# Hash-bucket attention and a routed MLP on one core: one tile of the first batch's tokens is routed, gathered and put through its expert ahead of the others

## The chip, the core and the metric

The kernel runs on one core of a Trainium2 chip, in one launch. The metric is the device time of the launch in microseconds (us), lower is better. In the text PE is TensorE, DVE is VectorE, ACT is ScalarE, POOL is GpSimd, and SP is SyncE, which here only issues transfers.

## What is computed

Three parts follow each other. Their inputs and outputs are f32.

```python
# attention: B, H, S, D = 2, 8, 768, 64; a key counts only if its 6 sign bits equal the query's
mask   = q_bucket[:, :, :, None] == k_bucket[:, :, None, :]
scores = where(mask, q @ k.T / 8, -1e9)
x      = softmax(scores) @ v              # -> x: N = 1536 tokens, 512 wide

# experts: each token goes to the one of E = 8 experts with the largest logit
logits = x @ w_gate + modality_bias[modality_id]
e_idx  = argmax(logits, axis=1)
for e in range(E):                        # w1[e]: 512 x 1024, w2[e]: 1024 x 512
    mask = e_idx == e
    out[mask] = gate_w[mask, None] * (maximum(x[mask] @ w1[e], 0) @ w2[e])

# last MLP: 512 -> 2048 -> 512 with softplus
return softplus(x @ w_in) @ w_out
```

How many tokens an expert gets depends on the data; the kernel must be right for any split.

## The kernel before

**Attention.** A *step* handles 128 queries of one head against all 768 keys, a *body* is 12 steps (two heads), and there are 8 bodies: body 0 and body 7 are written out on every engine, those between run in hardware loops (DVE also writes out body 4). Step u of a body does on PE the scores of step u + 2 (`scores`, L1183), a third of the values of an earlier group (`values`, L1208), at u = 1, 4, 7, 10 a fold of the finished group into the bank `ps7` (`fold_out`, L1219), and six transposes of the probabilities (L1195). DVE does the row maximum of step u + 2 (L848 with the read of its accumulator), at the fold steps the three operations of `normalise` (L864, L866, L869), and two subtractions `pTl` (L855) on what ACT has just rounded (L596). ACT also does the exponentials (L587). The order of each engine's work is written out by hand in these functions; engines meet at semaphores. POOL splits the next head's q, k and v (`split_qk`, `split_v`), SP loads heads and moves rows of bits. `x_ready` counts normalised groups of three steps, of 32; 16 of them are the first batch. `X` holds for each token and head 64 values and 8 partial logits; SP stores it to `x_rows` in DRAM (`store_x`).

**Routing.** After the last fold DVE adds the last partial logits and finds each token's expert (`onehot`, L939 to L944). PE ranks the tokens within their experts with small bf16 products of triangular and all-ones matrices (L1264 to L1272); DVE and POOL turn the ranks into a place, a tile and a lane; PE makes the source row of each sorted place (`source`, L1282) and its gate factor (L1287). POOL gathers 12 tiles of 128 rows from `x_rows` in sorted order with indirect transfers (L523); ACT multiplies by the gate (`gated`, L668), PE transposes (`turn_x`, L1298), DVE copies to `xT` (L1012). A table of tiles and tokens per expert is read into registers (L268).

**Experts.** Tiles of 128 tokens run expert by expert; a tile belongs to one expert, so partly filled tiles occur. In the loop a tile is split into a rounded part and a rest, as are the weights, and each product is three fp32r products: `w1_products` (24 matmuls of 512 columns, L1323), `turn_h` (8 transposes), `turn_y` (4, of the tile before), `w2_products` (24 of 512 columns, L1343 to L1347). Weights lie in a ring of two slots (`RING`); SP loads the next expert's w1 when the first layer of the last tile before it is done (`hB_done`), w2 when its second layer is (`y_done`). The first tile of all takes its first layer in plain f32 (`first_products`, L1305: 32 matmuls of 128 columns), since its split weights are not there yet:

```python
turn_x(0); first_products()
for n in range(1, TPB + 1): turn_x(n)
w2_products(0, 0)
for n in range(TPB + 1, TILES): turn_x(n)
for e in range(E):
    with nc.tensor.Fori(0 if e else 1, n_e) as i:
        w1_products(e, g); turn_h(g, 0); turn_y(g - 1); turn_h(g, 1); w2_products(e, g)
```

The last MLP follows and isn't touched.

## Time and profile before

| | us |
|---|---|
| median of 3 runs | 764.47 (763.66 to 765.12) |
| the profiled execution's own time | 764.26 |
| its span | 762.5 |
| PE / DVE / ACT / POOL busy | 727.0 / 573.2 / 499.1 / 316.3 |

Attention takes the first 251 us of the span, routing and the start of the experts last to 291, the loop over the expert tiles to 490, and the last MLP takes the rest. Busy shares count matmuls whose ends are modelled, so PE's 95% says only that it is seldom without an instruction. In the rows below L12 is line 12 of the kernel before; `x4` counts instructions in a row that were merged, and the bracket at a row's end tells how long the engine had been idle and what released it.

### The profile page before, as it was taken

The numbers are of one execution on the slowest core, as the hardware profiler recorded it, in microseconds if no ns is written. First come the engines' busy times: TensorE is split into PE (matmuls) and PEld (weight loads), VectorE is DVE, ScalarE is ACT, GpSimd is POOL, SyncE is SP. The second block draws the span as 40 slices with busy tenths as digits, with TensorE's granted clock in tenths as the row PEclk, the third lists the DMA queues.
The fourth block names the chain that finished last, engine by engine and source line by source line (L and its number), as shares of the span: only waits on it lengthen the run. The fifth ranks groups of instructions, "written<-read, shape, count | busy, mean of one in ns | idle before, by whom it ended". The sixth has DMA issues, their size and how long they took to land. (4 is left out here: it accounts for less than half of the span.)

```text
span 762.5 us, 13117 instructions
## 1 busy us (share of the span) xinstructions
PE 727.0 (95%) x3974; PEld 619.8 (81%) x3974; DVE 573.2 (75%) x915; ACT 499.1 (65%) x914; POOL 316.3 (41%) x277
## 2 busy tenths in 40 slices
PE   5999999999999399999999999999999999999996
PEld 4899898998999287888888888878887888878884
DVE  6989999999998566427996254298787888887884
ACT  6878888788887355527985363375656665666662
POOL 7767577666742440000000000055554745457543
PEclk9999999999999689999999999999999999999999
DMA  3763111311101242306896001033322433324321
GB/s 132 276 198 123 41 46 38 129 56 48 36 5 69 72 141 110 111 0 240 327 361 230 0 0 28 3 97 94 110 83 97 152 103 90 104 89 149 99 70 69
DMA packets 38879, 80.52 MB, mean 106 GB/s; under 512 B 5536, under 2 KB 9792, under 8 KB 38848
## 3 DMA queue, kind: packets, MB, share of 16 engines
q1 hardware_dynamic: 36208, 72.82, 28.9%
q0 software_dynamic: 1920, 6.69, 2.7%
q10 hardware_dynamic: 720, 0.64, 0.2%
q8 instruction: 15, 0.25, 0.1%
q14 instruction: 16, 0.13, 0.1%
HBM read 72.33 MB, written 6.68 MB: 104 GB/s over the span
## 5 line engine op out<-in xcount | busy, mean ns | idle before, releaser
L529 POOL TENSOR_TENSOR hres<-hexp,hres 128x512 f32<-128x512 f32 x46 | 59.7, 1297 | 320.1 <-DVE hres L1081 320.0
L596 ACT ACTIVATE pTh<-psA 128x384 fp32r<-128x384 f32 x192 | 83.9, 491 | 41.4 <-PE psA L1195 40.9
L855 DVE TENSOR_TENSOR pTl<-psA,pTh 128x384 fp32r<-128x384 f32 x192 | 97.9, 551 | 11.0 <-ACT pTh L596 9.7
L1183 PE MATMUL psA<-K,Q 128*128 128x384 f32 x384 | 93.2, 366 | 3.2 <-ACT K L633 1.6
L848 DVE TENSOR_SCALAR_CACHE_REDUCE psA<-psA 128x768 f32<-128x768 f32 x96 | 91.8, 957 | 3.4 <-PE psA L1183 3.4
L587 ACT ACTIVATE probs<-psA,negmax 128x768 f32<-128x768 f32 x96 | 87.4, 910 | 2.9 <-DVE psA L848 2.5
L1019 DVE SCALAR_TENSOR_TENSOR hTl<-psA,hTh 128x512 fp32r<-128x512 f32 x34 | 22.8, 689 | 87.5 <-ACT hTh L687 87.5
L1035 DVE TENSOR_TENSOR wil<-rawi,wih 128x512 fp32r<-128x512 f32 x48 | 79.1, 1650 | 6.5 <-ACT wih L707 6.5
L1195 PE MATMUL psA<-ident,probs 128*128 128x128 f32 x576 | 82.6, 279 | 1.1 <-DVE pTl L855 0.5
L765 ACT ACTIVATE habs<-psA 128x512 f32<-128x512 f32 x48 | 28.7, 597 | 77.8 <-PE psA L1396 77.8
L1195 PEld LDWEIGHTS psA<-ident,probs 128*128 128x128 f32 x576 | 65.0, 144 | 14.5 <-issue 5.9
L532 POOL TENSOR_TENSOR hsum<-hsum,hres 128x512 f32<-128x512 f32 x46 | 69.6, 1513 | 8.2 <-POOL hres L529 8.2
L1410 PE MATMUL psA<-woh,sh 128*128 128x512 f32 x184 | 72.2, 392 | 0.9 <-DVE sl L1098 0.7
L1412 PE MATMUL psA<-woh,sl 128*128 128x512 f32 x184 | 71.7, 390 | 0.0
L1411 PE MATMUL psA<-wol,sh 128*128 128x512 f32 x184 | 71.7, 389 | 0.0
L1183 PEld LDWEIGHTS psA<-K,Q 128*128 128x128 f32 x384 | 64.3, 195 | 6.2 <-issue 5.3
L1208 PE MATMUL ps<-pTh,vhl 128*128 128x384 f32 x186 | 62.7, 337 | 0.0
L1208 PE MATMUL ps<-pTl,vhl 128*128 128x384 f32 x186 | 62.6, 336 | 0.0
L1343 PE MATMUL ps<-w2h,hTh 128*128 128x512 f32 x136 | 54.9, 404 | 0.0
L1098 DVE TENSOR_TENSOR sl<-hsum,sh 128x512 fp32r<-128x512 f32 x47 | 53.6, 1141 | 0.9 <-ACT sh L779 0.9
L1344 PE MATMUL ps<-w2l,hTh 128*128 128x512 f32 x136 | 53.2, 391 | 0.0
L1396 PE MATMUL psA<-x2h,wih 128*128 128x512 f32 x192 | 51.7, 391 | 0.7 <-DVE hsum L1089 0.6
(185 smaller groups left out, 1653.5 us busy)
## 6 DMA issues: line engine op xcount, KB each, us to landing
w2s<-in_moe_w SPq DMA_DIRECT2D x8, 2048.0 KB, 9.3
w1s<-in_moe_w SPq DMA_DIRECT2D x8, 2048.0 KB, 9.4
rawi<-in_moe_w_in SPq DMA_DIRECT2D x48, 256.0 KB, 2.7
rawo<-in_moe_w_out SPq DMA_DIRECT2D x48, 256.0 KB, 2.8
raw<-in_qk SPq DMA_DIRECT2D x16, 384.0 KB, 3.1
vs<-in_v SPq DMA_DIRECT2D x16, 192.0 KB, 2.4
x_rows<-X SPq DMA_DIRECT2D x1, 1728.0 KB, 6.0
x_rows<-X SPq DMA_DIRECT2D x1, 1512.0 KB, 5.5
```

The source lines that it names most:

```text
L532: pool.tensor_tensor(hsum[u][:, :], hsum[u][:, :], hres[u][:, :], ALU.add).then_inc(s_done, 1)
L587: nc.scalar.activation(probs[u % 2][:, :].rearrange("p (a n) -> p a n", a=2), psA[u % 2][:, :, 0:HALF], ACT.Exp, bias=negmax[:, u % 4:u % ...
L596: nc.scalar.activation(pTh[u // TPGR % 2][:, g * TPH:(g + 1) * TPH, u % TPGR * P:(u % TPGR + 1) * P], psA[2][:, g, 0:HALF].rearrange("p (t ...
L848: V.tensor_scalar(psA[u % 2][:, :, 0:HALF], psA[u % 2][:, :, 0:HALF], PENALTY, PENALTY, ALU.min, ALU.min, accum_out=negmax[:, u % 4:u % 4 ...
L855: V.tensor_tensor(pTl[u // TPGR % 2][:, g * TPH:(g + 1) * TPH, cols], psA[2][:, g, 0:HALF].rearrange("p (t n) -> p t n", t=TPH), pTh[u // ...
L1035: V.tensor_tensor(wil[u][:, :, :], rawi[u][:, :, :], wih[u][:, :, :].bitcast(F32), ALU.subtract).then_inc(wi_split, 1)
L1183: last = T.matmul(psA[u % 2][:, h, 0:HALF], qs[par][:, cols], ks[par][:, h * HALF:(h + 1) * HALF], start=start, stop=not start)
L1195: last = T.transpose(psA[2][:, g, t * P:(t + 1) * P], probs[u % 2][:, kt * P:(kt + 1) * P], ident[:, :])
L1208: last = T.matmul(last_ps if type(G) is int and G == PAIRS - 1 else ps6[:, 0:COLS], vhl[gm // 2 % 2][:, kt, :], p[gm % 2][:, kt, :], start ...
L1410: T.matmul(acc[t], sh[u][:, cols], woh[u][:, :], start=first, stop=False)
L1411: T.matmul(acc[t], sh[u][:, cols], wol[u][:, :], start=False, stop=False)
L1412: last = T.matmul(acc[t], sl[u][:, cols], woh[u][:, :], start=False, stop=final)
```

## The change

In body 6 (`choose`) DVE finds the experts of the first batch's 768 tokens, counts them with one matmul of PE and takes the expert with most of them, `favourite`, and its number of tokens, at most 128. In body 7 (`collect`) it ranks the favourite's tokens with two matmuls, picks the first 128, and PE makes their source rows with 12 more. POOL gathers them (`xin0`), after it has summed the first batch's logits between bodies 4 and 5. SP loads the favourite's weights into slot 1 of the ring, which held expert 1's before; expert 1's weights are now loaded after this tile's products. The tile (tile 0) goes through both layers in plain f32: its first layer in three pieces between the routing's small products, its second between the transposes of the other tiles. The 128 tokens leave the regular sort; the favourite has 128 fewer. The first regular tile (tile 1) is now the one with a plain f32 first layer. Body 6 is written out on PE and DVE.

```diff
 # PE, attention
+                    if type(j) is int and j == BODIES - 2 and u == 6:
+                        pe.wait_ge(counts0_ready, 1)
+                        pe.wait_ge(x_ready, j * 4)
+                        T.matmul(ps7[:, 0:E], ones_b[:, :], sums16[:, 0, :], start=True, stop=True).then_inc(counts0_done, 1)
+                    if last and u == 3:
+                        pe.wait_ge(member_ready, 1)
...
+                    if last and u == 8:
...
                     if u % TPGR == 1 and not (first and u < 7):
+                        if type(j) is int and j == BODIES - 2 and u == 7:
+                            pe.wait_ge(counts0_read, 1)
+                        if last and u == 4:
+                            pe.wait_ge(rank0_read, 1)
+                        if last and u == 10:
+                            pe.wait_ge(source0_ready, 1)
```

```diff
 # DVE, attention: between row_max and low_pT of a step
+                    if type(j) is int and j == BODIES - 2:
+                        choose(u)
+                    if last:
+                        collect(u)
...
+                    elif u == 4:
+                        dve.wait_ge(rank0_done, 1)
+                        V.tensor_copy(rank0[:, :], ps7[:, 0:TPB]).then_inc(rank0_read, 1)
+                        dve.wait_ge(rank0_read, 1)
+                        alone(V.scalar_tensor_tensor(taken0[:, :], rank0[:, :], float(P), member[:, :], ALU.is_lt, ALU.mult))
...
+                    elif u == 6:
+                        V.scalar_tensor_tensor(pick0[:, :, :], iota_p[:, :].unsqueeze(1).broadcast_to([P, TPB, P]), 1.0,
+                                               over(key0[:, :], P), ALU.add, ALU.is_equal).then_inc(pick0_ready, 1)
...
+                    elif u == 11:
+                        dve.wait_ge(gathered_first, 16)
+                        alone(V.tensor_reduce(logit0[:, :], xin0[:, :, D:XROW].rearrange("p h e -> p e h"), AX.X, ALU.add))
```

```diff
 # SP
-                if i < 2 + 2 * RING:
-                    (load_w2, load_w1)[i % 2](i // 2 - 1)
+                if i < 4:
+                    (load_w2, load_w1)[i % 2](0)
...
+            sp.wait_ge(table0_ready, 1)
...
+            sp.dma_start(w1s[1][:, :, :], w1[bass.ds(at, 1)].rearrange("o (c p) f -> p (o c) f", p=P)).then_inc(w1_in[1], 16)
+            sp.dma_start(w2s[1][:, :, :], w2[bass.ds(at, 1)].rearrange("o (c p) f -> p (o c) f", p=P)).then_inc(w2_in[1], 16)
...
-            for e in range(RING, E):
...
+            for e in range(1, E):
...
                 sp.wait_ge(hB_done, before_e)
                 load_w1(e)
```

```diff
 # PE, start of the experts
+            pe.wait_ge(xT0_ready, 1)
+            pe.wait_ge(w1_in[1], 16)
+            first_layer(range(0, 2), w1s[1], xT0)
             pe.wait_ge(onehot_ready, 1)
...
             T.matmul(total_ps[:, 0:E], ones_b[:, :], sums16[:, 0, :], start=True, stop=True).then_inc(totals_done, 1)
+            first_layer(range(2, 6), w1s[1], xT0)
...
             last.then_inc(source_done, 1)
+            first_layer(range(6, FC), w1s[1], xT0)
...
-            turn_x(0)
-            pe.wait_ge(w1_in[0], 16)
-            pe.wait_ge(xT_ready, 1)
-            first_products()
...
-            for n in range(1, TPB + 1):
+            pe.wait_ge(w2_in[1], 16)
+            for n in range(5):
+                second_layer((n,))
                 turn_x(n)
-            w2_products(0, 0)
-            for n in range(TPB + 1, TILES):
-                turn_x(n)
+            second_layer(range(5, FC))
+            pe.wait_ge(w1_in[0], 16)
+            pe.wait_ge(xTf_ready, 1)
+            for f in range(FC):
+                first_layer((f,), w1s[0], xTf)
+                if f + 5 < TILES:
+                    turn_x(f + 5)
+            turn_y(0)
+            w2_products(0, 1)
```

`first_layer` does for each f four f32 matmuls of 128 columns, `second_layer` one f32 matmul of 512 columns. The order of the instructions shows it at two places.

PE, from the last fold to the first gathered tile, before (L1219 is the fold, L1264 to L1272 the ranks and counts, L1282 the source rows, L1287 the gates, L268 the table, L1298 `turn_x`, L1305 the first layer):

```order
L1219 MATMUL ps<-foldg,oT_102 128x72 x3
L1264 MATMUL psA<-onehot,before_b 128x96
...
L1272 MATMUL psA<-sums,ones_b 128x8
L1282 MATMUL psA<-carry,pick 128x12 x24
L1287 MATMUL psA<-gates,pick 128x36 x12
L268 TENSOR_LOAD table x2
L1298 MATMUL psA<-ident,xs_117 128x128 x4
L1305 MATMUL psA<-xT,w1s_49 128x128 x32
L1298 MATMUL psA<-ident,xs_118 128x128 x4
```

The same place now:

```order
L1464 MATMUL psA<-ident,xs_121 128x128 x4
L1397 MATMUL ps<-foldg,oT_102 128x72 x3
L1472 MATMUL psA<-xT_122,w1s_50 128x128 x8
L1490 MATMUL psA<-onehot,before_b 128x96
...
L1498 MATMUL psA<-sums,ones_b 128x8
L1472 MATMUL psA<-xT_122,w1s_50 128x128 x16
L1509 MATMUL psA<-carry,pick 128x12 x24
L1472 MATMUL psA<-xT_122,w1s_50 128x128 x8
L1515 MATMUL psA<-gates,pick 128x36 x12
L298 TENSOR_LOAD table x2
L1482 MATMUL ps<-w2s_54,hT_123 128x512
L1526 MATMUL psA<-ident,xs_117 128x128 x4
```

The 32 matmuls of tile 0's first layer (`xT_122` is `xT0`, `w1s_50` the ring's slot 1) stand around the ranks and the source rows, ahead of all gathered tiles; behind the table now comes tile 0's second layer (L1482), one matmul between each two transposed tiles.

DVE, steps 3 and 4 of body 7, now (L933, L949 to L954 and L940 are the former L848, L864 to L869 and L855):

```order
L933 TENSOR_SCALAR psA,negmax<-psA 128x2x384
L940 TENSOR_TENSOR pTl_82<-psA,pTh_94 128x3x128 x2
L933 TENSOR_SCALAR psA,negmax<-psA 128x2x384
L1044 COPY rank<-ps 128x6
L1046 SCALAR_TENSOR_TENSOR taken<-rank,member 128x6
L949 TENSOR_SCALAR den<-sums 128x3
L951 RECIPROCAL inv<-den 128x3
L954 TENSOR_TENSOR X<-ps,inv 128x3x72
L940 TENSOR_TENSOR pTl_82<-psA,pTh_94 128x3x128 x2
```

L1044 and L1046 are new; they stand behind the row maximum, and PE's fold of the same step waits for L1044 to have read `ps7`.

## Rows read from the trace of the kernel before

**Rows 1.** Stretches: length, busy us per engine, clock, DMA share, GB/s
```profile
195.00:222.00 27.00, 26.94 (x191) 24.39 (x191) 25.36 (x57) 22.42 (x51) 17.21 (x15) 1.00 0.05 13
222.00:249.00 27.00, 26.14 (x184) 25.08 (x183) 23.30 (x59) 19.87 (x46) 6.17 (x16) 1.00 0.16 59
```

**Rows 2.** Timeline of DVE, bodies 6 and 7: start us, us, instruction
```profile
208.63 0.55 DVE L864 TENSOR_SCALAR den<-sums 128x3 f32<-128x3 f32 x1
...
221.56 1.02 DVE L855 TENSOR_TENSOR pTl<-psA,pTh 128x384 fp32r<-128x384 f32 x2 [0.20 <-ACT pTh L596]
...
223.37 0.17 DVE L864 TENSOR_SCALAR den<-sums 128x3 f32<-128x3 f32 x1
```

**Rows 3.** DVE's groups by shape, 249 to 264: busy us, mean ns
```profile
L963 DVE TENSOR_TENSOR pick<-iota_p,lane_f 128x640 bf16<-128x640 f32 x2 | 1.8, 937 | 0.0
...
L939 DVE TENSOR_TENSOR lg<-lg,X 128x48 f32<-128x48 f32 x1 | 0.2, 209 | 0.1
...
L959 DVE SCALAR_TENSOR_TENSOR lane_f<-tile_f,place_f 128x12 f32<-128x12 f32 x1 | 0.2, 174 | 0.0
```

**Rows 4.** Timeline, step 4 of body 7: row maximum and fold
```profile
229.08 0.96 DVE L848 TENSOR_SCALAR_CACHE_REDUCE psA<-psA 128x768 f32<-128x768 f32 x1
229.10 0.78 PE L1219 MATMUL ps<-foldg,oT 128*128 128x72 f32 x6
```

**Rows 5.** Timeline: end of POOL split, PE near it, logit sums
```profile
160.77 1.85 POOL L452 TENSOR_TENSOR K<-raw,K 64x768 fp32r<-64x768 f32 x1 [0.34 <-POOL K L449]
...
169.77 0.51 PE L1183 MATMUL psA<-K,Q 128*128 128x384 f32 x2
...
243.99 3.08 POOL L507 TENSOR_TENSOR lg<-lg,X 128x96 f32<-128x96 f32 x7
```

**Rows 6.** Timeline from the ranks to the first tile's first layer
```profile
253.59 0.22 PE L1264 MATMUL psA<-onehot,before_b 128*128 128x96 bf16 x1 [2.30 <-DVE onehot L944]
...
258.21 0.81 PE L1282 MATMUL psA<-carry,pick 128*128 128x12 bf16 x22 [3.69 <-POOL carry L516]
...
262.67 0.54 PE L1287 MATMUL psA<-gates,pick 128*128 128x36 bf16 x12 [3.06 <-DVE gates L986]
...
264.65 0.72 ACT L668 ACTIVATE xs<-xin,gate_at 128x512 f32<-128x512 f32 x1 [8.77 <-DMA xin<-x_rows,source]
...
267.42 9.75 PE L1305 MATMUL psA<-xT,w1s 128*128 128x128 f32 x64 [0.88 <-DVE xT L1012]
```

**Rows 7.** Stretches, columns as in rows 1
```profile
269.00:271.00 2.00, 2.00 (x12) 2.00 (x11) 2.00 (x2) 2.00 (x2) 1.70 (x2) 0.50 0.85 240
...
273.00:275.00 2.00, 2.00 (x21) 2.00 (x20) 1.09 (x2) 0.60 (x1) 1.69 (x2) 1.00 0.34 106
```

**Rows 8.** Timeline: the last 20 records of L1305
```profile
274.77 2.40 PE L1305 MATMUL psA<-xT,w1s 128*128 128x128 f32 x20
```

**Rows 9.** PE reads the table: ns min/median/max, first and last start
```profile
L268 PEldq TENSOR_LOAD <-table x2: 345/431/517, 262.7 to 263.3; - x2
```

**Rows 10.** First product of the regular tiles, as rows 9
```profile
L1323 PE MATMUL psA<-w1h,xth x128: 387/389/476, 291.4 to 481.1; 128*128 128x512 f32 x128
```

**Rows 11.** Timeline of PE, regular tiles: turns, second layer, starts of two tiles
```profile
296.98 0.60 PE L1332 MATMUL psA<-ident,hrow 128*128 128x128 f32 x4
297.42 0.60 PE L1355 MATMUL ps<-ident,yrow 128*128 128x128 f32 x4
...
298.32 0.50 PE L1343 MATMUL ps<-w2h,hTh 128*128 128x512 f32 x1
...
303.89 1.07 PE L1323 MATMUL psA<-w1h,xth 128*128 128x512 f32 x4
...
316.26 1.07 PE L1323 MATMUL psA<-w1h,xth 128*128 128x512 f32 x4
```

**Rows 12.** Timeline of POOL: issue of the last of 12 gathers
```profile
277.03 0.95 POOL L523 DMA_INDIRECT xin<-x_rows,source  x1 [0.30 <-issue]
```

**Rows 13.** Stretches while one w1 loads, columns as in rows 1
```profile
301.00:303.00 2.00, 2.00 (x11) 1.65 (x10) 1.08 (x2) 2.00 (x2) 0.00 (x0) 1.00 1.00 410
```

More of the change, by code:

```diff
@@ L140, in build @@
         xs = [work(f"xs{i}", [P, DM], 99328 + 2048 * i) for i in range(2)]
+        pick0 = work("pick0", [P, TPB, P], 101376, BF16)
+        xin0 = work("xin0", [P, H, XROW], 99072)
+        xs0 = work("xs0", [P, DM], 101376)
+        xT0 = work("xT0", [P, DC, P], 103424)
+        hT0 = work("hT0", [P, FC, P], 105472)
+        xTf = work("xTf", [P, DC, P], 133120)
         w2h = work("w2h", [P, FC, DM], 0, F32R)
@@ L171, in build @@
         lower = sb("lower", [P, TILES, E])
-        at8 = sb("at8", [P, TILES, E])
+        at9 = sb("at9", [P, TILES, E + 1])
+        tok = sb("tok", [P, TPB, 2], BF16)
+        later = sb("later", [P, TPB, TPB])
+        member = sb("member", [P, TPB], BF16)
+        ahead_of = sb("ahead_of", [P, TPB], BF16)
+        rank0 = sb("rank0", [P, TPB])
+        taken0 = sb("taken0", [P, TPB])
+        key0 = sb("key0", [P, TPB])
+        chosen = sb("chosen", [P, E])
+        most = sb("most", [P, 1])
+        code0 = sb("code0", [P, 1])
+        table0 = sb("table0", [P, 2], I32)
+        source0 = sb("source0", [P, 1], I32)
+        logit0 = sb("logit0", [P, E])
+        neg0 = sb("neg0", [P, 1])
+        sum0 = sb("sum0", [P, 1])
+        gate0 = sb("gate0", [P, 1])
         highest = sb("highest", [P, TILES])
@@ L720, in _, with take_h0 @@
             nc.scalar.activation(tmp8[:, :, :], tmp8[:, :, :], ACT.Exp).then_inc(gexp_done, 1)
-            act.wait_ge(source_ready, 2)
-            for n in range(2):
-                gated(n)
+            def take_h0(half, done):
+                act.wait_ge(done, 1)
+                nc.scalar.activation(hT0[:, half * FC // 2:(half + 1) * FC // 2, :],
+                                     psA[1][:, half, :].rearrange("p (c n) -> p c n", c=FC // 2), ACT.Relu).then_inc(hT0_ready, 1)
+            take_h0(0, hA_done)
+            w1_high(0, 0)
+            take_h0(1, hB_done)
             act.wait_ge(table_ready, 1)
@@ L1251, in _ @@
             body(0, first=True)
-            with nc.tensor.Fori(1, BODIES - 1) as j:
+            with nc.tensor.Fori(1, BODIES - 2) as j:
                 body(j)
+            body(BODIES - 2)
             body(BODIES - 1, last=True)
@@ L1299, in turn_x @@
                 last.then_inc(xT_done, 1)
[L1301 to L1310 removed]
             def w1_products(e, g):
[L1314 removed]
+                pe.wait_ge(xl_ready, g - 1)
                 for half, done in ((0, hA_done), (1, hB_done)):
```

306 lines of the change are left out of this document (222 added, 84 removed).

## The prediction, written before the change was timed

> **What bounds the kernel now.** I read three things in this order. First the busy time by stretch in attention: DVE is busy 25.4 of 27 us in body 6 and 23.3 of 27 at the end [rows 1], more than ACT or POOL; PE's figure is no measure, since its ends are modelled. Then DVE's timeline, to see whether the rest is slack: in a step without a fold DVE does the row maximum, waits 0.20 us for ACT's `pTh` [rows 2] and goes on; steps with a fold or with bits show no such wait. So in attention nearly each us that DVE gets is a us on the path, less a gap of 0.2 in about half the steps. Third the timeline behind attention: PE does its ranks at 253.6, waits 3.7 us for `carry`, 3.1 for `gates`, and starts the first tile's first layer at 267.4 only [rows 6]. Its granted clock is at 0.50 (the 1.2 GHz level) when that layer starts and back at 1.00 from 273 us [rows 7]. The regular tiles start at 291.4 [rows 10], one each 12.37 us (303.89 to 316.26) [rows 11], with no stall seen in PE's rows.
>
> **1. One tile less in the loop: -12.4.** L1323 has 128 matmuls of `xth`, 8 in a tile, so 16 tiles are in the loop behind the one that is peeled [rows 10]. Now tile 0 and tile 1 stand ahead of it. The count of tiles stays at 17 if the favourite has 128 tokens in the first batch: taking a full tile from an expert takes one off its tiles. Counting the reference's choices on its own inputs, experts have 177, 484, 91, 35, 81, 7, 386 and 275 tokens, that is 2, 4, 1, 1, 1, 1, 4 and 3 tiles; expert 1 has 247 in the first batch, so it is the favourite, 128 are taken and 356 (3 tiles) stay. The loop then has 15: 12.37 us less.
>
> **2. Attention: +6.8.** DVE gets 16 operations in body 6 and 14 in body 7. Prices by size, from DVE's groups [rows 3]: 0.17 for one of a few elements, 0.21 for 48, and the `pick0` of 768 columns 1.07 (0.94 for 640, scaled with a fixed share of 0.27). Body 6: six of about 0.21, one count of 0.25 and nine small, 3.0 us. Body 7: 3.5 us, of which `pick0` is 1.07. Sum 6.5.
> - Off, what falls into the 0.2 us gaps: steps 0, 5, 6, 8 and 11 of body 6 and two of body 7, and both operations of step 11, where DVE no longer has a row maximum: -1.6.
> - On, the port: L864, which is small, takes 0.55 where POOL works and 0.17 where it doesn't [rows 2]. Four such (`tensor_scalar` and a cast between SBUF tiles) stand in steps 7, 9 and 10 of body 6, with POOL at work near all three: +1.0 (0 to 1.5).
> - On, a new wait in step 4 of body 7: the fold of that step went out at 229.10, just as the row maximum began at 229.08 (0.96 long) [rows 4]; now it needs `rank0_read`, behind that maximum and the copy: about 230.25. PE's transposes, ACT's rounding and DVE's `pTl` of the step are queued behind it. Of these 1.15 us the 0.3 of DVE's two operations are counted above: +0.85.
> The sum is 6.75. Bounds: 3.7 if all of DVE's idle time in the two bodies took operations in, 9.5 if none did and the waits between dependent operations came on top.
>
> PE's own additions (1, 2 and 12 matmuls of at most 8 columns) are hidden by its wait for `pTl`: the 24 like them at L1282 took about 1 us [rows 6], so 12 take 0.5 in step 8, where DVE has 0.38 to do at once. The gather of `xin0`: `source0` is ready in step 8 near 239.7, and after the routing it took 4.9 us from the end of L1282 (258.21, its last two included about 259.7) to ACT's start at 264.65 [rows 6]; that makes 244.6, DVE asks for it at 244.9. Hidden, 0.3 us ahead; if it is late, its lateness goes 1:1 onto the last step. The gate, `xs0` and its transposes fall in ACT's and PE's waits for the last values: 0.
>
> POOL's new place for bias and sums holds up the split for head 11 by some 5.4 us: seven sums of 96 columns took 3.08 [rows 5], those of 48 are put at 2.5, bias and constants at 2.9. It ended at 162.6 and would end at 168.0; PE's scores near it stand at 169.77 [rows 5]. Hidden, by 1.5 us at most. SP now waits for `table0` in front of nothing but the favourite's loads and the last stores: 0. Both loads, asked for near 219, are there by 235: 2 MB at 410 GB/s [rows 13] are 5 us.
>
> **3. From the gates to the loop: +1.8.** The first layer of tile 0 goes into PE's waits: 8 matmuls from 251.3 to 253.2 (ranks at 253.6), 16 to 258.2 (source rows at 258.2), 8 to 261.5 (gates at 262.7). A plain f32 matmul of 128 columns is two records of 0.117 (2.40 us for 20, less the last one's tail) [rows 8], 0.235. So 0 for it, if the clock stays at 1.00; the same work at 0.50 is a rival below. From the gates on PE has: the table, read at 262.7 and 263.3, 0.5 at most each, and a third read [rows 9], ready at 264.3; 8 f32 matmuls of 512 columns, 0.90 each (between 2 x 0.43 by columns and 4 x 0.235): 7.2; 12 turns of 0.44 (296.98 to 297.42) [rows 11]: 5.3; tile 1's first layer, 32 x 0.235: 7.5; `turn_y` 0.44; its second layer, 5.45 (298.32 to 303.89 less a start of 0.1) [rows 11]. Together 290.2, and 0.5 for the first gathered rows, which come at the pace of POOL's issue: 290.7. Before it was 291.4, so -0.7.
>
> Transfers come on top. Expert 1's w1 no longer lies in the ring; SP asks for it as soon as tile 0's first layer is done, near 262, in the midst of the 12 gathers. Before, the gathers alone took 0.85 of the DMA engines at 240 GB/s [rows 7], and one w1 alone takes all of them at 410 GB/s [rows 13]. If both share evenly, a gather takes 2.0 us in place of 1.25 until w1 is in at 275: `turn_x(4)` then waits till 273.6, not 271.1, and w2, asked for when tile 0's second layer is done, slows the last ones, which have 3 us in hand. I take +2.5, between 0 (gathers lose nothing) and 10 (weights go first).
>
> The Trainium skill (DMA: Bandwidth & Descriptors, "Issuing engines are not separate DMA queues") says that transfers from all engines run on the same 16 DMA engines and interleave. No stretch before has a gather beside a weight load, so no row shows how they share; by the rule the sum is the one below, without it 2.5 less.
>
> Sum: 764.26 - 12.4 + 6.8 + 1.8 = 760.5, against the profiled execution; the median of the runs lies 0.2 above it: **760.7**.
>
> **Rivals.**
> - *The cover is better* (the gaps take DVE's operations in, or the gathers lose nothing). Either alone gives -3 or -2.5, both 764.3 - 12.4 + 3.7 - 0.7 = 754.9; I price it 757. For it: POOL's last gather goes out at 277.0 [rows 12], 4 us before PE needs it now. Against: rows 2 show no gap in half the steps.
> - *Weights go first; slower.* The 2 MB of w1 pass ahead of gathers 1 to 5, 5.0 us at 410 GB/s [rows 13], and w2 ahead of the last ones, 5.0 less what is in hand: some 9.5 in place of 2.5, so 767.5. It decides from a third term of +7.2 on. For it: a load keeps the engines full with what is queued at once, while POOL feeds gathers one by one. Against: before, the gathers finished a while after their issue without trouble.
> - *The clock stays down.* At 0.50 the 16 matmuls behind the counts take 7.5, not 3.8, and hold up the source rows by 3.7, and the last 8 the gates by 0.8: 765.0, no change to be measured. For it: before, PE's clock fell in that very stretch [rows 6, 7]. Against: it fell while PE had hardly anything to do, and now it is to be busy.
>   The Trainium skill (TensorE: Matmul & The Clock Gate, Part 1) says "the default state is throttled, and activity releases the throttle", which speaks against this rival; the return to 1.00 in rows 7 agrees, the outcome here is shown by no run yet.
> - *No tile is saved* (the count above is wrong): 764.5 + 6.8 + 1.8 = 773.1, with a chance of 0.04.
>
> **How the numbers follow.** What a measurement of this kernel can tell from no change is 0.2%, 1.5 us. Chances: the forecast 0.50 (758 to 763.5 by its own bounds, a sixth of it above 762.9 and so "same"), better cover 0.20, weights first 0.16, clock 0.10, no tile 0.04. Faster 0.42 + 0.20 = 0.62; same 0.08 + 0.10 = 0.18; slower 0.16 + 0.04 = 0.20. The range 756.5 to 767 leaves out the low end of the second case, half of the third and all of the last.
>
> **What would show it.** Term 1: 120 records of `xth` in `w1_products` in place of 128, still 12.4 us apart. Term 2: the last fold's normalise ends 6.8 us later than at 251.8; steps without new work keep their length; the fold of step 4 in body 7 starts behind the copy from `ps7`. Term 3: the gates' matmuls at the same distance from the last fold, clock 1.00 throughout; the distance from the gates to the loop 30.5 us in place of 28.7, with waits of PE or ACT for `xin` in it. If the distance is under 29, transfers cost nothing; above 35, the weights go first. The prediction is wrong as a whole if attention grows by under 3 or over 10 us, or if POOL's split of head 11 is what the scores wait for.

## The result: 756.5 us, and the profile after

| | before | after |
|---|---|---|
| median (runs) | 764.16 us (4) | 756.48 us (4; 754.92 to 756.95) |
| ratio to before | | 0.9894, 95% interval 0.9876 to 0.9912 |
| profiled execution, its span | 764.26, 762.5 us | 756.76, 755.0 us |
| last normalise of attention starts | 251.39 | 253.10: **+1.7** |
| from there to the products for the gates | 11.28 | 11.11: -0.2 |
| from those to the first regular tile | 28.74 | 32.19: **+3.45** |
| first to last product of the regular tiles | 189.7 | 177.3: **-12.4** |
| behind it | 281.4 | 281.3: -0.1 |

The last five rows add up to the 7.5 us between the spans. 760.7 was forecast, and the range began at 756.5: the change saved 4.2 us more than forecast, and the median lies 0.02 us outside the range. Five more runs of the changed kernel (e15, below) had a median of 754.36, all nine together 755.4, so it is outside by more than that. In e15's profile attention grew by 1.0 us and the stretch from the gates to the first regular tile by 2.0: the rows of this table are of single executions.

What answers to [rows 10], the first product of the regular tiles (columns as there):

```profile
L1540 PE MATMUL psA<-w1h,xth x120: 389/389/389, 296.4 to 473.7; 128*128 128x512 f32 x120
```

120 records in place of 128: one tile less, and term 1 of the prediction stands to a tenth of a us.

PE behind attention and one row of ACT, to be read against [rows 6] (start us, us, engine, line, ...):

```profile
252.83 2.00 PE L1472 MATMUL psA<-xT,w1s 128*128 128x128 f32 x16
254.99 0.22 PE L1490 MATMUL psA<-onehot,before_b 128*128 128x96 bf16 x1 [0.16 <-DVE onehot L1122]
...
255.80 3.82 PE L1472 MATMUL psA<-xT,w1s 128*128 128x128 f32 x32
259.63 0.81 PE L1509 MATMUL psA<-carry,pick 128*128 128x12 bf16 x22
...
264.21 0.47 PE L1515 MATMUL psA<-gates,pick 128*128 128x36 bf16 x12 [1.30 <-DVE gates L1164]
265.83 1.10 PE L1482 MATMUL ps<-w2s,hT 128*128 128x512 f32 x2 [1.15 <-issue]
...
271.01 0.72 ACT L738 ACTIVATE xs<-xin,gate_at 128x512 f32<-128x512 f32 x1 [4.27 <-DMA xin<-x_rows,source]
271.78 1.11 PE L1526 MATMUL psA<-ident,xs 128*128 128x128 f32 x4 [3.48 <-ACT xs L738]
```

The waits of 3.69 and 3.06 us of [rows 6] are filled by the early tile's first layer. But a new wait stands behind the gates: PE's transposes of the second gathered tile begin after 3.48 us of idling, because ACT waits 4.27 us for that tile's rows. The stretches around it (columns as in [rows 1]):

```profile
269.00:271.00 2.00, 0.00 (x0) 0.00 (x0) 1.22 (x2) 0.00 (x0) 1.70 (x2) 1.00 1.02 411
271.00:273.00 2.00, 1.22 (x5) 1.22 (x6) 0.07 (x1) 1.16 (x2) 1.39 (x3) 0.64 1.04 404
273.00:275.00 2.00, 2.00 (x5) 0.86 (x5) 1.75 (x2) 1.53 (x3) 1.69 (x2) 0.51 1.04 394
275.00:277.00 2.00, 2.00 (x11) 1.22 (x10) 1.69 (x2) 1.05 (x2) 1.52 (x2) 1.00 0.96 302
```

The DMA engines are full until 275 (share 1.02 to 1.04, some 400 GB/s), and PE's granted clock, which had stayed at 1.00 through the routing, falls to 0.51 (the 1.2 GHz level) behind PE's idle stretch. What PE does from 271.78 to 275.11 (four transposes, two matmuls, four transposes) took 1.79 us in e1, at 1.00, and takes 3.33 here.

Attention grew by 1.7 us only. DVE in body 6, where 16 operations came in, and POOL's operation beside it:

```profile
207.09 2.12 POOL L465 TENSOR_SCALAR qs<-raw 64x768 f32<-64x768 f32 x1
208.61 0.63 DVE L1015 TENSOR_SCALAR chosen<-totals,most 128x8 f32<-128x8 f32 x1
208.74 0.51 DVE L949 TENSOR_SCALAR den<-sums 128x3 f32<-128x3 f32 x1
...
213.88 0.16 DVE L1019 TENSOR_REDUCE code<-chosen 128x1 f32<-128x8 f32 x1
213.96 0.14 DVE L1020 TENSOR_SCALAR most<-most 128x1 f32<-128x1 f32 x1
214.02 1.01 DVE L940 TENSOR_TENSOR pTl<-psA,pTh 128x384 fp32r<-128x384 f32 x2
```

Two things are to be seen. The three operations that don't wait for each other start 0.06 to 0.08 us apart, though the two small ones last 0.14 and 0.16. And the long one (0.63) ends at 209.24 with POOL's, which ran from 207.09 to 209.21; the existing `den` behind it, which had waited 0.55 in [rows 2], ends at the same time. The wait was met once, not twice.

Body 7, with PE's fold of step 4:

```profile
230.07 0.16 DVE L1044 COPY rank<-ps 128x6 f32<-128x6 f32 x1
...
230.29 0.89 PE L1397 MATMUL ps<-foldg,oT 128*128 128x72 f32 x6 [0.94 <-DVE rank L1044]
...
231.29 0.38 DVE L954 TENSOR_TENSOR X<-ps,inv 128x216 f32<-128x216 f32 x1 [0.56 <-PE ps L1397]
232.07 1.02 DVE L940 TENSOR_TENSOR pTl<-psA,pTh 128x384 fp32r<-128x384 f32 x2 [0.40 <-ACT pTh L659]
...
235.95 0.95 DVE L1051 SCALAR_TENSOR_TENSOR pick<-iota_p,key 128x768 bf16<-128x768 f32 x1
```

The fold of step 4 waits 0.94 us for the copy of the ranks, as forecast, and the selection matrix `pick0` takes 0.95.

### The profile page after: what moved, and what is told of

The parts are those of the page before. It is cut to its first block and busy times, and to the rows that moved or that the text cites. A ratio compares the mean times of both kernels' runs of the same rounds, so it can differ in the third digit from the quotient of the medians.

```text
span 755.0 us, 13130 instructions
## 1 busy us (share of the span) xinstructions
PE 726.8 (96%) x4017; PEld 618.0 (82%) x4017; DVE 573.3 (76%) x944; ACT 500.1 (66%) x916; POOL 318.3 (42%) x288
## 5 line engine op out<-in xcount | busy, mean ns | idle before, releaser
L659 ACT ACTIVATE pTh<-psA 128x384 fp32r<-128x384 f32 x192 | 83.9, 491 | 42.9 <-PE psA L1373 42.3
L940 DVE TENSOR_TENSOR pTl<-psA,pTh 128x384 fp32r<-128x384 f32 x192 | 97.8, 551 | 10.7 <-ACT pTh L659 9.6
L933 DVE TENSOR_SCALAR_CACHE_REDUCE psA<-psA 128x768 f32<-128x768 f32 x96 | 91.8, 956 | 2.6 <-PE psA L1361 2.5
L1560 PE MATMUL ps<-w2h,hTh 128*128 128x512 f32 x128 | 51.7, 404 | 0.0
L1617 PE MATMUL psA<-x2l,wih 128*128 128x512 f32 x192 | 51.4, 389 | 0.0
```

The lines of the kernel that those rows point to most:

```text
L659: nc.scalar.activation(pTh[u // TPGR % 2][:, g * TPH:(g + 1) * TPH, u % TPGR * P:(u % TPGR + 1) * P], psA[2][:, g, 0:HALF].rearrange("p (t ...
L933: V.tensor_scalar(psA[u % 2][:, :, 0:HALF], psA[u % 2][:, :, 0:HALF], PENALTY, PENALTY, ALU.min, ALU.min, accum_out=negmax[:, u % 4:u % 4 ...
L940: V.tensor_tensor(pTl[u // TPGR % 2][:, g * TPH:(g + 1) * TPH, cols], psA[2][:, g, 0:HALF].rearrange("p (t n) -> p t n", t=TPH), pTh[u // ...
L1617: last = T.matmul(hps[u], w[u][:, d, :], x[:, d, g * GTOK:(g + 1) * GTOK], start=first, stop=(w is wil and d == DC - 1))
```

## The experiments

Since single spans scatter by 1 us and more, each run is read in two ways: the median and its ratio to the kernel before on the same chip, and distances inside the profiled execution, which repeat to 0.07 us where nothing was touched (body 6 of the changed kernel: 29.34 to 29.41 in the nine runs that leave it and the bodies ahead of it alone). *Body 6* is the distance from its first row maximum to that of body 7; *body 7* from there to the last normalise of attention (the row maximum stands two steps ahead of its own step, in all kernels); *gates to loop* as in the table above.

| kernel | median us | ratio to before, interval | body 6 | body 7 | gates to loop |
|---|---|---|---|---|---|
| before | 764.16 | | 29.62 | 31.05 | 28.74 |
| changed | 756.48 | 0.9894 (0.9876 to 0.9912) | 29.39 | 32.69 | 32.19 |
| e15: changed, again | 754.36 | 0.9880 (0.9864 to 0.9896) | 29.37 | 32.70 | 30.76 |
| e1: load behind the gathers | 752.16 | 0.9853 (0.9836 to 0.9870) | 29.36 | 32.69 | 27.64 |
| e2: ranks in step 3 | 754.74 | 0.9878 (0.9864 to 0.9893) | 29.37 | 31.96 | 32.13 |
| e3: before, body 6 written out | 762.70 | 0.9985 (0.9976 to 0.9993) | 29.27 | 31.04 | 28.50 |
| e4: 16 products more | 762.24 | 0.9978 (0.9966 to 0.9991) | 36.33 | 34.85 | 31.04 |
| e5: 16 maxima more | 759.35 | 0.9938 (0.9924 to 0.9951) | 31.64 | 33.71 | 32.31 |
| e6: DVE's bodies written out | 756.26 | 0.9886 (0.9870 to 0.9901) | 29.47 | 32.68 | 33.38 |
| e7: `pick0` on POOL | 754.72 | 0.9880 (0.9865 to 0.9895) | 29.34 | 32.67 | 30.79 |
| e8: e1, first layer behind the gates | 759.20 | 0.9930 (0.9917 to 0.9944) | 29.36 | 32.71 | 35.46 |
| e9: e1 + e2 | 751.30 | 0.9830 (0.9817 to 0.9844) | 29.35 | 32.02 | 27.66 |
| e10: e9 + bodies written out | 751.10 | 0.9829 (0.9816 to 0.9842) | 29.43 | 31.98 | 27.65 |
| e11: e9 + `pick0` on POOL | 752.44 | 0.9843 (0.9829 to 0.9856) | 29.36 | 32.25 | 27.64 |
| e12: all four | 750.93 | 0.9826 (0.9812 to 0.9839) | 29.46 | 32.10 | 28.54 |
| e13: e9, only the copy in step 3 | 751.95 | 0.9836 (0.9823 to 0.9849) | 29.41 | 31.48 | 29.19 |
| e14: e13 + bodies written out | 750.35 | 0.9817 (0.9804 to 0.9829) | 29.44 | 31.49 | 28.57 |
| e16: before, bodies written out | 762.75 | 0.9976 (0.9966 to 0.9986) | 29.28 | 31.07 | 28.52 |

### e1: does the load of expert 1's w1 hold up the gathers?

```diff
                 sp.wait_ge(hB_done, before_e)
+                if e == 1:
+                    sp.wait_ge(gathered[TILES - 1], 16)
                 load_w1(e)
```

> The changed kernel, but SP asks for expert 1's w1 only when the last of the 12 gathers has landed. Theory (the loads share the DMA engines with the gathers, and this is what the second gathered tile waits for): in the changed kernel ACT waits 4.27 us for xin at 271.0, PE 3.48 us behind it, and PE's clock falls to 0.51 to 0.64 for 2 to 3 us behind that wait. All this goes: gates to loop 28 to 28.5 us in place of 32.2, so 3.5 to 4.5 us faster than the changed kernel, near 752.4. Rival (the gathers land late by themselves, since rows are scattered or POOL issues them slowly): gates to loop stays within 0.5 us of 32.2 and the time is the same. Second rival (the load is only moved, to where its wait is met again, at expert 1's first tile): gathers early, but a wait of ACT for w1 in the loop, no gain.

27.64 us from gates to loop, and 4.3 us off the median against the first four runs of the changed kernel (2.2 against e15's, where the intervals of the ratios still touch; the 3.1 to 4.5 us between the profiles carry the reading). The stretch in e1 (columns as in [rows 1]), and PE there:

```profile
269.00:271.00 2.00, 2.00 (x8) 0.77 (x6) 2.00 (x4) 1.07 (x2) 1.70 (x2) 1.00 0.80 221
271.00:273.00 2.00, 1.76 (x9) 0.95 (x9) 2.00 (x3) 1.71 (x3) 1.54 (x2) 1.00 0.70 212
```
```profile
272.77 0.63 PE L1528 MATMUL psA<-ident,xs 128*128 128x128 f32 x4 [0.24 <-DVE xT L1192]
```

The wait of 3.48 is gone, the clock stays at 1.00, and the loads, now asked for at 281.7 and 282.1, are there long before expert 1 begins (ACT splits its w1 at 300.4 with no wait). The theory holds, both rivals fall. Of the 4.5 us between the two profiles, 3.5 are the wait and 1.5 the slower clock behind it, less the shorter waits that e1 has. How the two shared the DMA engines shows in the queues of the changed kernel (q1 is SP's load, q0 POOL's gathers: packets, MB, share), first from 265 to 267 us, then from 269 to 271; the last row is e1's from 265 to 267, without the load:

```profile
q1 hardware_dynamic: 175, 0.72, 87.8%
q0 software_dynamic: 34, 0.08, 11.2%
```
```profile
q1 hardware_dynamic: 104, 0.43, 52.5%
q0 software_dynamic: 106, 0.40, 49.8%
```
```profile
q0 software_dynamic: 113, 0.38, 71.2%
```

For the first 4 us the load took seven parts in eight (from 267 to 269 it was 171 packets against 29), then half. The gathers had more to move: POOL had begun to send off three by 265, as in e1, where 113 packets of theirs passed in the same 2 us. The Trainium skill (DMA: Bandwidth & Descriptors, "Queues, rings and completion order") says that a DMA engine takes turns between the queues it has work for, a packet at a time. The second stretch agrees with that, 104 packets against 106; the first doesn't, 175 against 34.

### e2, e9 and e13: the new wait in step 4

```diff
-                    elif u == 4:
+                    elif u == 3:
                         dve.wait_ge(rank0_done, 1)
                         V.tensor_copy(rank0[:, :], ps7[:, 0:TPB]).then_inc(rank0_read, 1)
```

The comparison `taken0` behind the copy moves with it. In e13, which has e1's edit too, it goes back to step 4 and only the copy stays.

> The changed kernel, but DVE reads the ranks from PSUM in step 3 of body 7, not in step 4. Theory (the fold of step 4 waits for that read, and all queued behind it on PE): the fold starts near 229.2 in place of 230.29, the last normalise of attention ends 0.8 to 1.2 us earlier, the time is 0.8 to 1.2 us below the changed kernel. Rival (the step waits for ACT or the row maximum anyway, and the late fold is caught up): less than 0.3 us. Second rival (the read in step 3 waits for PE's rank product, which ends near 227.25, and delays that step): slower by 0.1 to 0.5.

> The changed kernel with both edits at once: expert 1's w1 asked for behind the gathers (e1), and the ranks read in step 3 (e2). Alone they gave 4.3 us and 1.7 us of medians against the changed kernel, of the latter 0.75 us inside body 7. Theory (two separate stretches, nothing shared): 0.6 to 1.5 us faster than e1, so 750.7 to 751.5. Rival (the gates come earlier but the gathers don't, and PE waits for them): the same as e1, 752.2.

> e9, but only the copy of the ranks out of PSUM stands in step 3; the comparison of 6 columns behind it goes back to step 4. In e2, e9 and e10 that comparison took 1.00 to 1.02 us in step 3, since it began within 0.01 us of POOL's split of V (227.98 and 227.97 in e9) and ended with it. Theory (that wait is what it costs): the comparison takes 0.16 to 0.2 us, attention ends 0.6 to 0.9 us earlier than in e9, near 750.6. Rival (step 3 has slack, or ACT's pTh ends last there): within 0.2 us of e9, 751.3.

From row maximum to row maximum, steps 3 and 4 of body 7 took 2.11 and 2.63 us before, 2.18 and 3.81 in the changed kernel, 2.94 and 2.50 in e2, 2.14 and 2.66 in e13. So the late fold had cost 1.18 us. e2 took it away and paid 0.76 of it again, for an operation on 6 columns: body 7 is 0.73 us shorter, just under the 0.8 to 1.2 of its theory, and its median, 754.74, lies between the two of the changed kernel, so as a time it shows nothing. e9 is 0.9 us below e1, as its theory has it, with runs that overlap. Here is the comparison in e9, with POOL's operation:

```profile
227.97 1.01 POOL L510 TENSOR_TENSOR vhl<-vs,vhl 128x384 fp32r<-128x384 f32 x1 [0.18 <-POOL vhl L508]
```
```profile
227.78 0.16 DVE L1046 COPY rank<-ps 128x6 f32<-128x6 f32 x1
227.98 1.02 DVE L1048 SCALAR_TENSOR_TENSOR taken<-rank,member 128x6 f32<-128x6 f32 x1
228.93 1.01 DVE L942 TENSOR_TENSOR pTl<-psA,pTh 128x384 fp32r<-128x384 f32 x2
```

The comparison began 0.01 us behind POOL's split of V and ended with it. In e13 the comparison takes 0.16:

```profile
229.46 0.16 DVE L1049 SCALAR_TENSOR_TENSOR taken<-rank,member 128x6 f32<-128x6 f32 x1
229.54 0.16 DVE L951 TENSOR_SCALAR den<-sums 128x3 f32<-128x3 f32 x1
```

Body 7 is 0.54 us shorter than in e9, near the forecast of 0.6 to 0.9. The median isn't: 751.95 against 751.30. e13's profile lost 1.5 us from gates to loop, 1.14 of it in one wait of PE for a gathered tile. The local theory holds; as a time, e13 is no gain over e9.

### e3 and e16: what does a loop cost DVE?

```diff
-            with nc.vector.Fori(BODIES // 2 + 1, BODIES - 1) as j:
+            with nc.vector.Fori(BODIES // 2 + 1, BODIES - 2) as j:
                 body(j, 1)
+            body(BODIES - 2, 1)
             body(BODIES - 1, 1, last=True)
```

> The kernel before, but DVE's body 6 is written out behind the loop, as the changed kernel has it, with no new operation in it. Theory (in a loop the column of X that a fold's normalise writes comes from a register, and DVE starts that instruction 0.14 to 0.28 us later behind the reciprocal than with a constant: 0.34 to 0.46 us from start to start in body 6 of before, 0.21 in the changed kernel; four folds): 0.7 to 1.1 us faster than before, so that 16 small operations of body 6 in the changed kernel cost about 0.7 us and not 0. Rival (the gap behind the reciprocal is slack, since ACT's pTh comes no sooner): within 0.2 us of before, and then the 16 operations are free.

> The kernel before with all of DVE's bodies 1 to 6 written out, and nothing else. Theory (a register in the address of a fold's normalise delays it by 0.14 to 0.28 us, four times in a body; body 6 alone gave 1.46 us of medians, 0.5 of it in its own profile): 2 to 4 us faster than before, 760.5 to 762.5. Rival (body 6 alone has all of the gain, the rest is hidden behind ACT and PE): 762.5 to 763.

A fold's last operations in body 6, before (first fence) and in e3:

```profile
201.83 0.18 DVE L866 RECIPROCAL inv<-den 128x3 f32<-128x3 f32 x1
202.17 0.38 DVE L869 TENSOR_TENSOR X<-ps,inv 128x216 f32 x1 [0.16 <-DVE inv L866]
```
```profile
201.43 0.17 DVE L866 RECIPROCAL inv<-den 128x3 f32<-128x3 f32 x1
201.64 0.38 DVE L869 TENSOR_TENSOR X<-ps,inv 128x216 f32<-128x216 f32 x1
```

In the loop, with a register in the address, 0.34 us pass from start to start here and 0.34 to 0.46 in the four folds of the body; written out, with a constant, 0.21. (The edit takes the whole loop away; that it is the address isn't shown apart.) Body 6 becomes 0.35 us shorter, less than the 0.8 of the four gaps together, so part of them had been slack. The median is 1.46 us lower (the ratio 0.15%), more than the profile shows inside the body, and the rest of it isn't explained here. With all bodies written out (e16) the median is no lower than with one, 762.75, where 2 to 4 us had been forecast; the ratios, 0.9976 against 0.9985, leave room for some 0.7 us. What this says of the changed kernel: its body 6 is written out too, and 29.39 against e3's 29.27 is the net price of its 16 operations: **0.13 us** (0.06 to 0.14 over the runs that repeat either body).

The rows of the two traces show where the rest went. Six of the 16 stand in fold steps, ahead of a `den` that waits for POOL anyway: from the end of the row maximum to the end of `den` the four folds take 2.6 us in e3 and 2.8 in the changed kernel. The other ten filled most of DVE's waits for ACT's `pTh`: 1.19 us in e3's body 6, 0.14 in the changed kernel's.

### e4 and e5: 16 operations more

Behind each operation of `choose` one more, on constants, into a tile that nobody reads; e4 a product, e5 a maximum. The edit of e5:

```diff
+                for n in range({6: 2, 9: 2, 10: 3}.get(u, 1)):
+                    alone(V.tensor_reduce(spare[n][:, :], first_tile(by_tile(iota_e[:, :])), AX.X, ALU.max))
```

> The changed kernel with 16 more small DVE operations in body 6: behind each that chooses the expert one product of 48 columns on constants, into a tile that nobody reads (the kernel's outputs don't change). Theory (a small operation that doesn't wait for the one ahead starts 0.06 to 0.12 us behind it, and the wait for the port that POOL shares is met once in a step whatever the number): +1.0 to +1.9 us. Rival as in the prediction (0.21 us each, and more where POOL works): +3.4 us or more. Second rival (the steps have slack): under 0.4 us.

> The changed kernel with 16 more small DVE operations in body 6 at the same places as in e4_double_small, but maxima of 48 into 6 columns in place of products (into tiles that nobody reads, the outputs don't change). In e4 DVE's products that began while POOL ran an operation ended with it, up to 1.81 us later. Theory (what an added operation costs is 0.1 us from start to start, less the slack of its step; the 5.8 us of e4 were waits for the end of POOL's running operation, which a maximum over columns doesn't make): +0.2 to +1.5 us against the changed kernel, and none of the added maxima longer than 0.25 us. Rival (any operation shifts the steps against POOL's and the existing ones then wait): +3 us or more, with the waits in the operations that were there. Second rival (fixed price of 0.2 us each): +3.2 us with no long operation.

e4's body 6 grew by 6.9 us, twice the 3.4 at which its dearest case began, body 7 by 2.2, and the median by 5.8 to 7.9. The longest wait in it, POOL and DVE:

```profile
202.31 1.82 POOL L492 TENSOR_TENSOR Q<-qs,Q 64x768 fp32r<-64x768 f32 x1 [0.18 <-POOL Q L489]
```
```profile
202.38 1.81 DVE L1005 TENSOR_TENSOR onehot<-first,red 128x48 bf16<-128x48 f32 x1
```

The operation that waited longest was none of the added ones, but an operation of the change, moved to where POOL had just begun (added products waited too, one for 0.88 us at 199.78). In e5 no added maximum waited: alone they take 0.19 to 0.25 us. Through step 9, with 12 of them, e5's row maxima fell back by 0.33 us against the changed kernel, 0.03 each. Then this:

```profile
216.08 1.82 POOL L492 TENSOR_TENSOR Q<-qs,Q 64x768 fp32r<-64x768 f32 x1 [0.18 <-POOL Q L489]
```
```profile
216.24 1.68 DVE L950 TENSOR_SCALAR den<-sums 128x3 f32<-128x3 f32 x1
```

In the changed kernel `den` of that step began 0.17 us ahead of the same operation of POOL and took 0.15; here it begins 0.16 behind it. Step 10 grew by 1.6 us with it, and the five behind it by 1.4 more, in part waits of DVE for ACT (0.68 in the first of body 7); the median is 2.9 to 5.0 us up. So my theory for e5 (that kinds of operation which don't wait would settle it) falls, and its rival holds: it matters where the existing ones end up. The Trainium skill (SBUF — State Buffer, "SBUF: two separate sides") has the rule: DVE and GpSimd share a pair of ports that is an exclusive lock. A GpSimd operation takes it, and so does a DVE operation in a two-port mode or with two inputs in SBUF; the one that starts first has it for its whole instruction, and the other is blocked. Each pair of rows here agrees, with ends within 0.1 us of each other (204.13 and 204.19; 217.90 and 217.92; 228.98 and 229.00).

### e6, e10, e12, e14: DVE's bodies 1 to 5 written out

```diff
-            with nc.vector.Fori(1, BODIES // 2) as j:
-                body(j, 0)
-            body(BODIES // 2, 1)
-            with nc.vector.Fori(BODIES // 2 + 1, BODIES - 2) as j:
-                body(j, 1)
+            for j in range(1, BODIES - 2):
+                body(j, 1 if j >= BODIES // 2 else 0)
```

> The changed kernel with DVE's bodies 1 to 5 written out too, so that DVE has no loop in attention and no register in an address or a wait there. Writing out body 6 alone made the kernel before 1.46 us faster (0.35 of it seen inside that body). Theory (each body in a loop costs 0.35 to 1.1 us more): -1.8 to -5 us against the changed kernel, that is 751.5 to 754.7. Rival (what e3 gained was a shift in the start of attention that differs from build to build): within 1 us of the changed kernel. Second rival (the longer program is fetched more often and DVE waits for code): slower.

> e9 with DVE's bodies 1 to 5 written out as well. In e6 attention ended 1.5 us earlier than in the changed kernel, and the distance from the gates to the loop was 33.4 us in place of 32.2, so that nothing was left of it; there the gathers shared the DMA engines with the load. Theory (the loss was the load's; without it attention's gain stays): 0.5 to 1.5 us faster than e9. Rival (what attention gained was its early start, which differs from execution to execution by 0.5 to 0.9 us, and writing out bodies 1 to 5 gains nothing): within 0.4 us of e9.

> e11 with DVE's bodies 1 to 5 written out as well: all four edits. Theory (they add): 0.5 to 1.5 us faster than e11, near 749.5. Rival: as for e10, within 0.4 us of e11.

> e13 with DVE's bodies 1 to 5 written out. Theory (the two add, and bodies 1 to 5 give what the profiles of e6, e10 and e12 showed, 1.4 us): 1.0 to 1.6 us faster than e13, near 749.3. Rival (medians of e6 and e10 stood only 0.2 below their counterparts): within 0.4 us of e13.

Against their counterparts the medians moved by -0.2 (e6, first runs) or +1.9 (e6, e15's), -0.2 (e10), -1.5 (e12) and -1.6 us (e14); in the profiles body 6 began 0.8 to 1.6 us earlier in all four. Two things are mixed in that. From the first row maximum of body 1 to that of body 6 it is 147.0 to 147.4 us in all kernels with loops and 146.3 to 146.5 in the five without (e16 too): 0.7 to 1.0 us are the loops'. Where body 1 begins scatters from 42.9 to 44.0 whatever the kernel, and the rest is that. In the medians the gain shows in e12 and e14 and not in e6 and e10, so as a time it is likely but not certain. Behind the gates PE's clock fell to 0.50 in e12 (265 to 267) and e14 (264 to 266), with no load beside the gathers: e12's stretch to the loop is 0.9 us longer than e11's, e14's is 0.6 shorter than e13's, which had waited for a gathered tile. e14 has the lowest median of the study; its interval overlaps those of e9, e10 and e12.

### e7 and e11: the selection matrix on POOL

```diff
 # POOL
+            pool.wait_ge(key0_ready, 1)
+            for t in range(TPB):
+                pool.tensor_scalar(pick0[:, t, :], iota_p[:, :], 1.0, key0[:, t:t + 1],
+                                   ALU.add, ALU.is_equal).then_inc(pick0_ready, 1)
...
 # DVE, step 6
-                        V.scalar_tensor_tensor(pick0[:, :, :], iota_p[:, :].unsqueeze(1).broadcast_to([P, TPB, P]), 1.0,
-                                               over(key0[:, :], P), ALU.add, ALU.is_equal).then_inc(pick0_ready, 1)
```

> The changed kernel, but the selection matrix of the early tile is built by POOL in 6 pieces of 128 columns, not by DVE in one operation of 0.95 us in step 6 of body 7. Theory (POOL is idle there and DVE is on the path): step 6 shrinks by 0.65 us, the last normalise of attention ends 0.5 to 0.7 us earlier. Rival (POOL's pieces of about 0.6 us each, 3.6 in all, come too late for PE's product in step 8, and PE waits, or DVE's small operations wait for them): 0 to 2 us slower.

> e9 with the selection matrix built by POOL in 6 pieces, as in e7, but from ranks that are there a step earlier. In e7 step 6 became 0.65 us shorter, and steps 8 and 9 longer by 0.5, since POOL's pieces took 4.24 us and PE's product of step 8 came late. Theory (a step more of room hides POOL's pieces): 0.4 to 0.9 us faster than e9. Rival (DVE's small operations of the fold in step 4 or 7 then meet POOL at work and wait for its piece, 0.7 us at a time): within 0.3 us of e9, or slower.

In e7 step 6 went from 2.75 to 2.11 us, and steps 7 and 8 from 2.51 and 2.00 to 2.63 and 2.40: body 7 is unchanged (32.67). e7's rows say why:

```profile
233.56 4.24 POOL L564 TENSOR_SCALAR pick<-iota_p,key 128x128 bf16<-128x128 f32 x6 [5.09 <-DVE key L1052]
239.28 0.45 PE L1426 MATMUL ps<-tok,pick 128*128 128x1 bf16 x12
240.16 0.88 ACT L663 ACTIVATE pTh<-psA 128x384 fp32r<-128x384 f32 x2 [0.65 <-PE psA L1375]
240.68 1.02 DVE L944 TENSOR_TENSOR pTl<-psA,pTh 128x384 fp32r<-128x384 f32 x2 [0.32 <-ACT pTh L663]
```

POOL's pieces end at 237.80, 1.5 us before PE's 12 products of step 8, and these stand at the same distance from the start of body 7 as in the changed kernel: so they don't come late, though the text for e11 says so. What ends step 8 is ACT's `pTh`, which waits 0.65 us for PE's transposes behind the products (0.30 in the kernel before, without products). In the changed kernel `pick0` on DVE and the products on PE lie side by side, so taking one away gives nothing. Theory and rival of e7 both fall in their mechanism. e7's median, 754.72, lies between the two of the changed kernel, and no gain is shown. In e11 body 7 is 0.23 us longer than in e9, so the rival has the outcome; but no operation of DVE in e11 is drawn out by one of POOL's pieces (231.04 to 235.29), which was its mechanism.

### e8: what are the filled waits worth?

On PE the three pieces of the early tile's first layer become one behind the gates; on ACT expert 0's w1 is split first, and the layer's two halves are rounded behind the second gathered tile.

```diff
...
-            first_layer(range(6, FC), w1s[1], xT0)
             pe.wait_ge(gates_ready, 1)
...
             last.then_inc(source_done, 1)
+            pe.wait_ge(xT0_ready, 1)
+            pe.wait_ge(w1_in[1], 16)
+            first_layer(range(0, FC), w1s[1], xT0)
```

> The kernel of e1_load_after_gathers, but the first layer of the early tile (32 products, 7.5 us) stands on PE behind the products for the gates, not in three pieces ahead of the ranks, the source rows and the gates; ACT splits expert 0's w1 before it. Theory (the three pieces fill waits of PE and cost nothing there): gates at the same place or up to 0.5 us earlier, gates to loop 33 to 36 us in place of 27.6, 5 to 8 us slower than e1. Rival (behind the gates PE has waits for the first gathered rows that this work fills as well): less than 3 us slower. For PE's clock: the pieces keep it at 1.00 in e1; without them it falls to 0.50 between ranks and gates as in the kernel before, if what it did there was what held it.

```profile
259.26 0.82 PE L1509 MATMUL psA<-carry,pick 128*128 128x12 bf16 x22 [3.71 <-POOL carry L581]
...
263.87 0.54 PE L1514 MATMUL psA<-gates,pick 128*128 128x36 bf16 x12 [3.20 <-DVE gates L1168]
264.24 10.09 PE L1476 MATMUL psA<-xT,w1s 128*128 128x128 f32 x64
```

7.8 us more from gates to loop than in e1, 7.0 in the median, so the theory holds: the waits of [rows 6] are back, the clock is at 0.50 from 257 to 269, and the layer takes 10.09 us in place of 7.9 in three pieces (2.00, 3.82, 2.03). The gates stand where they stood (11.14 us behind the last normalise, 11.11 in e1), so in the changed kernel the pieces cost nothing there.

### e15: the changed kernel again

> The changed kernel, unchanged, for more runs on this chip: 756.5, by the runs so far 754.9 to 757.0. If its median is under 755.5, the gains of e2 and e7 against it were partly scatter.

Its runs went from 754.16 to 756.66. In this profile gates to loop took 30.76 us, PE waited 1.72 for the second gathered tile, and the clock was at 0.50 from 266 to 268 instead, ahead of that wait. All kernels without e1's edit lie between 30.76 and 33.38 there, those with it (and the pieces in place) between 27.64 and 29.19. Two things vary in these stretches, when the gathered rows come and where the clock falls. By e15's runs the gains of e2 and e7 against the first four runs (1.7 and 1.8 us) were partly scatter, as feared.

## Why the prediction was wrong

The sum was to be 764.26 - 12.4 + 6.8 + 1.8 = 760.5; the profiled execution had 756.76. Two terms were off, and in opposite directions: attention by 5.1 us too much, the stretch behind the gates by 1.7 too little (0.2 more came off between them). The forecast is only 4 us out because they partly cancel, which was luck. Step by step:

- **Term 1, one tile less, -12.4: right**, 120 records and 12.4 us.
- **Term 2, attention, +6.8: this step failed**; it was +1.7 (+1.0 in e15): body 6 began 0.3 later, was 0.2 shorter, and body 7 was 1.6 longer. What failed is the price of the added operations. Its parts:
  - The operations, 6.5 by full durations, less 1.6 for gaps. Measured: the 16 of body 6 cost 0.13 us against a body 6 written out without them (e3), 12 more cost 0.33 (e5). For body 6 the sum had 3.0 for durations, 1.0 off for gaps and 1.0 on for the port. The gaps were right: 1.05 us of waits for ACT were filled. A duration was the wrong price: it counts the tail that lies beside the next operation, and what DVE loses is the distance from start to start, 0.06 to 0.12 us for those that wait for nothing (e5's 12 maxima: some 2.4 us by durations, 1.4 from start to start, 0.33 on the path). And the waits for POOL, put down as a cost, were room: six of the operations stand ahead of a `den` that waits anyway, and cost 0.2 together. In body 7 step 6 grew by 0.65 with `pick0`, less than its 1.07, and even that isn't what it cost, since e7 takes it away and body 7 stays as long.
  - The port, +1.0: right as a mechanism, with nearly none of that sum, since in steps 4, 7 and 10 the existing `den` had made the same wait already. But it was bounded by 1.5 us for all, and e4 shows 6.9 for 16 operations more. The change's operations happen to lie well.
  - The new wait, +0.85 and 1.15 with the two operations themselves: right. Step 4 grew by 1.18 us, and 0.7 to 1.2 of body 7 come back with an earlier read (e2, e13).
  - Left out: that writing out body 6 for its constants gains by itself, 0.35 us in the body, 1.46 in the median of e3.
  - The hidden ones mostly were: body 6 began 0.3 us later than before, in e15 0.4 earlier. POOL's split for head 11 ended at 168.4 (168.0 forecast), and the early tile's rows were there when DVE asked. PE's 12 products were not: ACT waits 0.35 us more behind them, and in the changed kernel `pick0` covers that.
- **Term 3, gates to loop, +1.8: undersized**, 3.45 in this profile and 2.0 in e15's. What e1 leaves, 27.64, is 0.4 below the 28.0 worked out without transfers. The load's share is then 3.1 to 4.5 us, not 2.5 (of the profiles; late rows and a fallen clock cost up to 1.5 without it, e13 and e12), because it took seven eighths of the engines at first, and because PE's clock fell behind the wait.
- **The rivals.** "The cover is better" had the right half: it gave 757 and 0.20. "Weights go first" was nearer in mechanism than an even share, and had the wrong price, 9.5 us, by counting w2 too, which is asked for at 280.5, when the late gathers no longer hold PE up. The clock stayed up through the routing for the reason given, since PE had work (e8 is the counterpart); it fell in another place.
- **The range** leaned on 3.7 as the least for attention. Its lower bound let all of DVE's idle time take operations in at their full durations, and so was no bound. The text named the test itself: wrong as a whole if attention grows by under 3.

## What to carry to other kernels

Price a small operation beside others by the distance of starts in the trace, not by its duration, and take off the waits that it fills, for whatever engine: an operation ahead of one that waits anyway costs next to nothing, as long as it doesn't push that one into the next wait (e5). Then look at which operation of POOL runs there, since on DVE one of 3 to 48 columns can cost nothing or 1.0 to 1.8 us, and moving it by a step decides. Where a change frees a buffer earlier, ask what transfer that starts, and let the load that isn't needed yet wait for the transfers that are: one wait on SP gave 2 to 4 us here. Of the versions tried, e14 (that wait, the ranks copied a step earlier, DVE's bodies written out) has the lowest median, 750.35 us, 0.9817 of before.

## What the runs showed of the hardware that I had not expected

- A load and the gathers beside it did not share evenly from the start: 0.72 MB against 0.08 in 2 us, where the gathers alone moved 0.38 in e1, then 0.43 against 0.40.
- A DVE operation on 48 columns took 1.81 us beside a POOL operation of 1.82, and an operation that was there before can be pushed into such a place by a shift of 0.33 us against POOL's (0.15 to 1.68 for the same `den`, from 0.17 ahead of POOL's start to 0.16 behind it).
- In a hardware loop, with a register in the address of one operand, a DVE operation came 0.13 to 0.25 us later than written out (0.34 to 0.46 against 0.21 from start to start, four folds). Five bodies written out were 0.7 to 1.0 us shorter together.
- The same kernel, without any change, had its granted clock down from 271 to 275 in one execution and from 266 to 268 in another. Ahead of the first PE had been idle for 3.5 us, ahead of the second for all but 0.47 of 2.9 us (262.15 to 265.06).
